# Routing rounds by six digit steps in place of nine, with equal keys settled by running counts

## The chip, the cores and the metric

The kernel runs on one core of a Trainium2 chip, in one launch, in fp32 at its inputs and its output. The time is the device time in microseconds of that core; the number given for a kernel is the median over its runs. A core has five engines that work side by side: TensorE (PE in the profile) for matrix products, VectorE (DVE) and ScalarE (ACT) for elementwise work, GpSimd (POOL), and SyncE (SP), which starts transfers.

## The reference

Three stages follow one another on 2304 tokens of 512 values: attention, a routed layer with eight experts, and a rational function between two matrix products. The routing is the part of interest:

```python
def _moe_ref(x, w_gate, w1, w2):
    ...
    cap = N // E                      # 288
    logits = x @ w_gate               # 2304 x 8
    order = np.argsort(-logits.flatten())
    ...
    for idx in order:
        tok, e = (int(idx) // E, int(idx) % E)
        if assigned[tok] >= 0 or counts[e] >= cap:
            continue
        assigned[tok] = e
        counts[e] += 1
    ...
        h = np.maximum(x[mask] @ w1[e], 0.0)
        out[mask] = h @ w2[e]
```

Pairs of a token and an expert are taken in falling order of their logit, each token once, until an expert has 288 tokens. Each expert's network then runs on its own 288 tokens.

## The kernel before

The tokens lie as 128 partitions by NT = 17 columns, so that `logit` is 128 x 17 x 8. Attention fills `logit` in its last part. The routing (`routing_dve`, `routing_pe`) is a loop of seven rounds, written with `Fori(0, E - 1)`, and a pass behind it for the tokens that are left. In each round every free token has a best open expert (`choice`, one-hot) and a `key`, its logit there. At least one expert is closed in each round: the round looks for the largest key at which some open expert has as many tokens at or above it as it still has places (`need8`), and gives these tokens away.

The key is searched by digits, from the highest. A float key is turned into an integer in the same order (`flip`, L777 to L781), cut into seven digits (L772), and the token's number, in three more digits of which one is shared with the key's last bits, makes all keys different; these are nine digits `digit[:, 0:9, :]`, with 32 values each and 16 in the last. A digit step is:

- VectorE compares `y`, the scaled remainder of the key, with the values 1 to k of `kval`: `ge`, 128 x k x 18 in bf16, in two halves of 10 and 8 columns (L805).
- TensorE counts: for each of the 17 columns, a product of `choice` (128 x 8, the weights) with `ge[:, 0:k, t]` (128 x k, read with a stride of 18 elements), added up in `pO` (L862). The first half of `ge` releases ten of the products, the second seven.
- Beside it VectorE makes `w` and `z`, the next remainder (L808, L811).
- VectorE compares the counts with `need8`: `sat`, 8 x k (L815). TensorE adds up `sat` over the experts: `pX` (L865). VectorE counts the values with a sum above 0.5: `found`, the digit (L818), and makes the next `y` from `z` and `found` (L821).

Behind the last step VectorE marks the tokens at or above the key (`took`, L822; `new`, L823), sums them by expert (`newsum`, L827), updates `free` and `owner`, TensorE adds the sums over the partitions in two products (L867, L868), and VectorE updates `room`, `closed` and `need8` (L832 to L838). The next round begins with `opened` (L736), `keys` (L733), `is_best` (L740), then `ranked`, `first_rank`, `is_first` (L744 to L751), which leave the first of several equal experts, and `chosen` (L755).

The order on an engine is the order of the program. `do` counts an instruction on the semaphore `s_rt`, `after(k)` makes VectorE wait for the k-th, and `link` does both at once: a linked instruction ends before the next starts.

```python
                def link(ins):
                    after(do(ins))
```

GpSimd works beside the routing: it subtracts the high parts of `w_in` and `w_out` from their originals (L919, four instructions of 2048 elements each, as soon as transfers have landed) and does the same with the first expert's weights (L1028). Then it waits for `slot`, the place of each token, and scatters the tokens' rows to memory, sorted by expert (L885, 17 indirect transfers). SyncE loads the first expert's rows behind that, and the experts' part begins. Ahead of everything, `routing_setup_pool` and `routing_setup_dve` make the constants; VectorE's attention work stands behind the latter.

## Time and profile before

| | us |
|---|---|
| time, median of 3 runs | 1251.15 (1249.8 to 1251.74) |
| the profiled execution | 1253.45 |
| its span, first to last instruction | 1251.6 |
| attention, to the last logit | 0 to 279 |
| routing, to the last `slot` | 279 to 523 |
| scatter, loads and first products | 523 to 560 |
| experts and rational function | 560 to 1252 |
| PE / DVE / ACT / POOL busy in the span | 965.1 / 792.7 / 506.8 / 244.9 |

The profile is of one execution, and its own time is 1.85 us above its span. The granted TensorE clock is 0.9 of full speed in the attention and the experts' part and 0.5 in the routing. In the timelines a row gives the start and the length in us, the engine, the line, the operation with output and inputs, and in brackets the idle time ahead of it and what ended it. An instruction's length includes the time that it stands still for a resource. Successive instructions of an engine overlap a little, by some 0.08 us on VectorE.

### The profile page before, as it was taken

How to read it: one execution, taken by the hardware profiler on the slowest of the kernel's cores; microseconds unless marked ns; L12 is line 12 of the kernel's file. 1: busy time of each engine (PE TensorE's matmuls, PEld its weight loads, DVE VectorE, ACT ScalarE, POOL GpSimd, SP SyncE). 2: the span in 40 equal slices, each digit the busy share in tenths (PEclk: the TensorE clock that was granted, in tenths of full speed). 3: DMA queues.
4: the chain of work that ended last, by engine and by line, in shares of the span. 5: the costliest groups of instructions: out<-in, count | busy, mean ns of one | idle time of the engine just before them, and what ended most of it. 6: DMA issues, size and time to landing. Idle time of an engine off the chain costs nothing.

```text
span 1251.6 us, 22365 instructions
## 1 busy us (share of the span) xinstructions
PE 965.1 (77%) x7769; PEld 895.3 (72%) x7769; DVE 792.7 (63%) x1757; ACT 506.8 (40%) x1108; POOL 244.9 (20%) x199
## 2 busy tenths in 40 slices
PE   5999999972133444219899898998998988989994
PEld 4888888851123333219899898998998988988994
DVE  4555554438876666403975966939849759488484
ACT  3555555520010000003744735627547457266362
POOL 2000000005530000230421412313215114132101
PEclk9999999975555555559999999999999999999998
DMA  7622222204320000135015024051060240420200
GB/s 224 191 64 64 64 64 64 46 11 134 135 67 0 0 0 0 52 130 154 1 39 132 0 75 96 0 135 36 17 154 0 67 103 0 110 61 0 69 1 18
DMA packets 106280, 80.62 MB, mean 64 GB/s; under 512 B 72016, under 2 KB 88400, under 8 KB 105232
## 3 DMA queue, kind: packets, MB, share of 16 engines
q1 hardware_dynamic: 97184, 62.83, 19.1%
q0 software_dynamic: 9072, 17.47, 4.5%
q8 instruction: 15, 0.25, 0.1%
q14 instruction: 9, 0.07, 0.0%
HBM read 70.94 MB, written 9.31 MB: 64 GB/s over the span
## 4 chain that ended last, share of the span: by engine, by line
PE 51%; DVE 35%; issue 7%; ACT 3%; POOL 2%; DMA 1%; DVEq 0%; ACTq 0%; SPq 0%; POOLq 0%
PE pS L1095 6%; PE pS L1097 6%; PE pS L1096 6%; DVE num L1351 6%; DVE num L1353 6%; PE pO L862 5%; PE pS L339 4%; DVE den L1340 3%; DVE num L1344 3%; PE pO L362 3%; DVE ge L805 2%; PE pO L363 2%; DVE num L1342 2%; DVE den L1349 2%; DVE z L811 2%
## 5 line engine op out<-in xcount | busy, mean ns | idle before, releaser
L1028 POOL TENSOR_TENSOR w_lo<-w_raw,w_hi 128x512 fp32r<-128x512 f32 x80 | 129.8, 1643 | 290.8 <-ACT w_hi L1023 290.8
L1023 ACT ACTIVATE w_hi<-w_raw 128x512 fp32r<-128x512 f32 x80 | 45.5, 616 | 275.9 <-DMA w_raw<-in_moe_w 275.9
L1095 PE MATMUL pS<-x_hi,win_hi 128*128 128x272 f32 x512 | 149.2, 292 | 4.5 <-DVE num L1344 4.5
L862 PE MATMUL pO<-ge,choice 128*8 128x32 bf16 (+1 forms) x1071 | 71.1, 233 | 101.6 <-DVE ge L805 101.6
L1097 PE MATMUL pS<-x_hi,win_lo 128*128 128x272 f32 x512 | 148.0, 289 | 0.0
L1096 PE MATMUL pS<-x_lo,win_hi 128*128 128x272 f32 x512 | 147.9, 289 | 0.0
L862 PEld LDWEIGHTS pO<-ge,choice 128*8 128x8 bf16 x1071 | 59.2, 102 | 108.5 <-DVE ge L805 108.5
L1095 PE MATMUL pT<-g_hi,wout_hi 128*128 128x272 f32 x256 | 79.5, 310 | 47.0 <-DVE g_lo L1331 47.0
L1095 PEld LDWEIGHTS pS<-x_hi,win_hi 128*128 128x128 f32 x512 | 96.4, 188 | 6.6 <-DVE num L1344 6.3
L1096 PEld LDWEIGHTS pS<-x_lo,win_hi 128*128 128x128 f32 x512 | 96.4, 188 | 0.0
L1097 PEld LDWEIGHTS pS<-x_hi,win_lo 128*128 128x128 f32 x512 | 96.3, 188 | 0.0
L1095 PEld LDWEIGHTS pT<-g_hi,wout_hi 128*128 128x128 f32 x256 | 49.8, 195 | 55.0 <-issue 54.6
L1351 DVE SCALAR_TENSOR_TENSOR num<-num,coef,habs 128x544 f32<-128x544 f32 x64 | 86.1, 1345 | 0.0
L1353 DVE SCALAR_TENSOR_TENSOR num<-den,num 128x544 f32<-128x544 f32 x64 | 80.4, 1256 | 2.2
L1395 POOL DMA_INDIRECT out<-orow,number x32 | 37.6, 1175 | 214.2 <-DVE orow L1375 206.8
L485 ACT ACTIVATE prob<-pS,negmax 128x224 f32<-128x224 f32 x128 | 55.8, 444 | 55.9 <-DVE negmax L521 55.4
L1095 PE MATMUL pS<-x_hi,w_hi 128*128 128x272 f32 x256 | 76.1, 297 | 1.2 <-POOL w_lo L1028 1.2
L1096 PE MATMUL pT<-g_lo,wout_hi 128*128 128x272 f32 x256 | 75.6, 295 | 0.0
L1097 PE MATMUL pT<-g_hi,wout_lo 128*128 128x272 f32 x256 | 75.5, 295 | 0.0
L1097 PE MATMUL pS<-x_hi,w_lo 128*128 128x272 f32 x256 | 75.1, 293 | 0.0
L1258 ACT ACTIVATE g_hi<-num 128x544 fp32r<-128x544 f32 x64 | 42.3, 660 | 80.9 <-DVE num L1353 76.3
L1096 PE MATMUL pS<-x_lo,w_hi 128*128 128x272 f32 x256 | 74.9, 292 | 0.0
(222 smaller groups left out, 2851.8 us busy)
## 6 DMA issues: line engine op xcount, KB each, us to landing
...
```

The costliest lines, as they stand in the source:

```text
L339: last = nc.tensor.matmul(bank[:, h * KW:(h + 1) * KW], qT[par][:, h, i * P:(i + 1) * P], kT[par][:, i, :], start=False, stop=True, skip_g ...
L485: e = nc.scalar.activation(prob[:, i, h, :], pS[:, i * 512 + h * KW:i * 512 + (h + 1) * KW], ACT.Exp, bias=negmax[par][:, c:c + 1], accum_ ...
L862: last = nc.tensor.matmul(pO[0:E, 0:k], choice[:, t, :], ge[:, 0:k, t], start=t == 0, stop=t == NT - 1)
L1023: nc.scalar.activation(piece(w_hi, slot, k % 2), piece(w_raw, slot, k % 2), ACT.Copy).then_inc(s_whi, 1)
L1028: nc.gpsimd.tensor_tensor(piece(w_lo, slot, k % 2), piece(w_raw, slot, k % 2), piece(w_hi, slot, k % 2).bitcast(F32), ALU.subtract).then_i ...
L1095: nc.tensor.matmul(dst, hi, x_hi, start=start, stop=False)
L1096: nc.tensor.matmul(dst, hi, x_lo, start=False, stop=False)
L1097: return nc.tensor.matmul(dst, lo, x_hi, start=False, stop=stop)
L1258: nc.scalar.activation(g_hi[k % 2][:, :, :], num[k % 2][:, :, :], ACT.Copy).then_inc(s_gh, 1)
L1351: nc.vector.scalar_tensor_tensor(n, n, coef[:, 0:1], r, ALU.add, ALU.mult).then_inc(s_ratio, 1)
L1353: nc.vector.scalar_tensor_tensor(n, d, 2.0, n, ALU.subtract, ALU.mult).then_inc(s_g, 1)
L1395: nc.gpsimd.indirect_dma_start(out, bass.IndirectOffsetOnAxis(number[:, s:s + 1].bitcast(U32), 0), orow[s][:, :], None).then_inc(s_send, 16)
```

## The change

The key is cut into six digits, of 64, 64, 32, 32, 32 and 32 values, and the token's number is no longer part of it. `y` is fp32 in place of bf16 and always scaled by 64; with it `z` needs one addition (the passes `w` are gone). Keys can now be equal at the end. So each round marks the tokens above the key (`above`) and those equal to it (`tied`), both in `won`, laid out by expert; TensorE makes the sum of those above, the sum of all, and, with the triangular matrix `before`, how many equal ones lie in lower partitions, in five products; a running count over each expert's columns (`tensor_tensor_scan` into `spot`) then says which of the equal ones still find a place. Another running count (`count`) finds the first of several equal experts of a token, in place of `ranked`, `first_rank` and `is_first`. The token's being free comes from `owner` (`holding`, `lifted`) in place of `free`. `kval` has 64 values in place of 32. The experts' and the attention's parts are untouched.

```diff
-        KG = 32
-        DIGITS = [(27, 31), (22, 31), (17, 31), (12, 31), (7, 31), (2, 31), (0, 3)]
-        LD = len(DIGITS)
-        KS = [KG] * 8 + [16]
-        ND = len(KS)
-        IDMAX = 4095
+        DIGITS = [(26, 63), (20, 63), (15, 31), (10, 31), (5, 31), (0, 31)]
+        KS = [m + 1 for _, m in DIGITS]
+        ND = len(DIGITS)
+        KG = max(KS)
+        RADIX = float(KG)
         ABOVE = 1e6
...
-        took = sb("took", [P, NT], BF16)
-        new = sb("new", [P, NT, E], BF16)
-        newsum = sb("newsum", [P, E], BF16)
+        y = sb("y", [P, NT + 1])
+        won = sb("won", [P, 2, E, NT + 1])
+        wonsum = sb("wonsum", [P, 2, E], BF16)
...
-            nc.gpsimd.iota(erank[:, :], pattern=[[-1, E]], base=E, channel_multiplier=0,
-                           allow_small_or_imprecise_dtypes=True).then_inc(s_const, 1)
+            nc.gpsimd.memset(fresh_e[:, :, :], 1.0).then_inc(s_const, 1)
...
-        TSETUP = 13
+        TSETUP = 9
...
-            link(nc.vector.tensor_scalar(flip[:, :], token[:, :], -1.0, float(IDMAX), ALU.mult, ALU.add))
-            link(nc.vector.tensor_scalar(tokbits[:, 0, :], flip[:, :], 9, None, ALU.logical_shift_right))
-            link(nc.vector.tensor_scalar(tokbits[:, 1, :], flip[:, :], 4, 31, ALU.logical_shift_right, ALU.bitwise_and))
-            link(nc.vector.tensor_scalar(tokbits[:, 2, :], flip[:, :], 15, None, ALU.bitwise_and))
-            link(nc.vector.memset(dconst[:, :, :], 1 / KG))
-            link(nc.vector.tensor_scalar(dconst[:, LD - 1:ND, :], tokbits[:, :, :], 1.0, 1 / KG, ALU.add, ALU.mult))
+            link(nc.vector.memset(fresh_e[:, :, 0:1], 0.0))
+            link(nc.vector.memset(fresh_t[:, :, :], 1.0))
+            link(nc.vector.memset(fresh_t[:, :, 0:1], 0.0))
             link(nc.vector.memset(y[:, :], 0.0))
-            link(nc.vector.tensor_copy(digit[:, LD:ND, :], dconst[:, LD:ND, :]))
-            link(nc.vector.memset(free[:, :], 1.0))
+            link(nc.vector.memset(won[:, :, :, :], 0.0))
             link(nc.vector.memset(room[:, :], float(CAP)))
             link(nc.vector.memset(closed[:, :], 0.0))
             link(nc.vector.memset(room8[:, :], float(CAP)))
             link(nc.vector.memset(need8[:, :], float(CAP)))
...
+            def holding():
+                return nc.vector.tensor_reduce(out=held[:, :], in_=owner[:, :, :], axis=AX, op=ALU.add)
+
+
+            def lifted():
+                return nc.vector.scalar_tensor_tensor(lift[:, :], held[:, :], -FULL, key[:, :], ALU.mult, ALU.add)
+
...
-                                               key[:, :].unsqueeze(2).to_broadcast([P, NT, E]), ALU.is_equal)
...
+                                               lift[:, :].unsqueeze(2).to_broadcast([P, NT, E]), ALU.is_equal)
+
+
+            def counted():
+                return nc.vector.tensor_tensor_scan(count[:, :, :].rearrange("p t e -> p (t e)"),
+                                                    fresh_e[:, :, :].rearrange("p t e -> p (t e)"),
+                                                    best[:, :, :].rearrange("p t e -> p (t e)"), 0.0, ALU.mult, ALU.add)
 
             def chosen():
-                return nc.vector.tensor_tensor(choice[:, :, :], best[:, :, :],
-                                               free[:, :].unsqueeze(2).to_broadcast([P, NT, E]), ALU.mult)
+                return nc.vector.scalar_tensor_tensor(choice[:, :, :], count[:, :, :], 1.0, best[:, :, :], ALU.is_equal,
+                                                      ALU.mult)
...
-                link(opened())
...
+                    shift, m = DIGITS[j]
+                    return nc.vector.tensor_scalar(digit[:, j, :].bitcast(I32), flip[:, :], shift, m, ALU.logical_shift_right,
+                                                   ALU.bitwise_and)
+
+                k_open = do(opened())
+                k_held = do(holding())
+                after(k_open)
+                k_key = do(keys())
+                after(k_key)
                 k_sign = do(nc.vector.tensor_scalar(flip[:, :], bits, 31, -2 ** 31, ALU.arith_shift_right, ALU.bitwise_or))
-                after(k_best)
-                k_ranked = do(ranked())
+                k_lift = do(lifted())
                 after(k_sign)
                 k_flip = do(nc.vector.tensor_tensor(flip[:, :], bits, flip[:, :], ALU.bitwise_xor))
-                after(k_ranked)
-                k_rank = do(first_rank())
+                after(k_lift)
+                k_best = do(is_best())
                 after(k_flip)
-                do(cut(0))
-                do(cut(1))
-                after(k_rank)
-                k_first = do(is_first())
-                do(cut(2))
-                do(cut(3))
-                after(k_first)
+                for j in range(3):
+                    do(cut(j))
+                after(k_best)
+                k_count = do(counted())
+                for j in range(3, ND):
+                    k_cut = do(cut(j))
+                after(k_count)
                 do(chosen())
-                do(cut(4))
-                do(cut(5))
-                link(cut(6))
-                link(nc.vector.scalar_tensor_tensor(digit[:, 0:LD, :], dbits[:, :, :], 1 / KG, dconst[:, 0:LD, :], ALU.mult,
-                                                    ALU.add))
-
-
-
-                link(nc.vector.tensor_scalar(y[:, 0:NT], digit[:, 0, :], float(KG), None, ALU.mult))
+                after(k_cut)
+                link(nc.vector.tensor_scalar(digit[:, :, :], digit[:, :, :].bitcast(I32), 1 / RADIX, 1 / RADIX, ALU.mult, ALU.add))
+
+
+
+                link(nc.vector.tensor_scalar(y[:, 0:NT], digit[:, 0, :], RADIX, None, ALU.mult))
                 for j in range(ND):
                     k = KS[j]
                     for t0, t1 in ((0, HALF), (HALF, NT + 1)):
                         nc.vector.tensor_tensor(ge[:, 0:k, t0:t1], y[:, t0:t1].unsqueeze(1).to_broadcast([P, k, t1 - t0]),
                                                 kval[:, 0:k, t0:t1], ALU.is_ge).then_inc(s_ge, 1)
-                    if j > 0:
-                        link(nc.vector.tensor_scalar(w[:, :], z[:, :], found[:, :], None, ALU.subtract))
-                    y_now = w[:, :] if j > 0 else digit[:, 0, :]
                     if j < ND - 1:
-                        link(nc.vector.scalar_tensor_tensor(z[:, :], y_now, float(KG), digit[:, j + 1, :], ALU.mult, ALU.add))
-                    else:
-                        link(nc.vector.tensor_scalar(z[:, :], y_now, float(KG), None, ALU.mult))
+                        link(nc.vector.tensor_tensor(z[:, :], y[:, 0:NT], digit[:, j + 1, :], ALU.add))
                     dve.wait_ge(s_cnt, ph * ND + (j + 1))
...
                     link(nc.vector.tensor_scalar(anyk[:, 0:k], pX[:, 0:k], 0.5, None, ALU.is_gt, ALU.add,
                                                  accum_out=found[:, :]))
                     if j < ND - 1:
-                        link(nc.vector.tensor_scalar(y[:, 0:NT], z[:, :], found[:, :], float(KG), ALU.subtract, ALU.mult))
-                link(nc.vector.scalar_tensor_tensor(took[:, :], z[:, :], found[:, :], free[:, :], ALU.is_ge, ALU.mult))
-                link(nc.vector.tensor_tensor(new[:, :, :], choice[:, :, :], took[:, :].unsqueeze(2).to_broadcast([P, NT, E]),
-                                             ALU.mult))
-
+                        link(nc.vector.tensor_scalar(y[:, 0:NT], z[:, :], found[:, :], RADIX, ALU.subtract, ALU.mult))
+                    else:
+                        link(nc.vector.tensor_scalar(z[:, :], y[:, 0:NT], found[:, :], None, ALU.subtract))
+
+
+                past = z[:, :].unsqueeze(2).to_broadcast([P, NT, E])
+                above = won[:, 0, :, 1:NT + 1].rearrange("p e t -> p t e")
+                tied = won[:, 1, :, 1:NT + 1].rearrange("p e t -> p t e")
+                k_above = do(nc.vector.scalar_tensor_tensor(above, past, 0.5, choice[:, :, :], ALU.is_gt, ALU.mult))
+                k_tied = do(nc.vector.scalar_tensor_tensor(tied, past, 0.0, choice[:, :, :], ALU.is_equal, ALU.mult))
+                after(k_tied)
                 with nc.allow_low_precision("counts up to NT"):
-                    nc.vector.tensor_reduce(out=newsum[:, :], in_=new[:, :, :].rearrange("p t e -> p e t"), axis=AX,
-                                            op=ALU.add).then_inc(s_took, 1)
-                do(nc.vector.tensor_tensor(free[:, :], free[:, :], took[:, :], ALU.subtract))
-                do(nc.vector.tensor_tensor(owner[:, :, :], owner[:, :, :], new[:, :, :], ALU.add))
+                    nc.vector.tensor_reduce(out=wonsum[:, :, :], in_=won[:, :, :, 1:NT + 1], axis=AX, op=ALU.add)\
+                        .then_inc(s_took, 1)
+                k_owner = do(nc.vector.tensor_tensor(owner[:, :, :], owner[:, :, :], above, ALU.add))
                 dve.wait_ge(s_count, ph + 1)
-                k_room = do(nc.vector.tensor_tensor(room[:, :], room[:, :], pT[0][:, 0:E], ALU.subtract))
+                k_lim = do(nc.vector.tensor_tensor(won[:, 1, :, 0], pT[0][:, 0:E], room[:, :], ALU.subtract))
+                after(k_lim)
+                k_scan = do(nc.vector.tensor_tensor_scan(spot[:, :, :].rearrange("p e t -> p (e t)"),
+                                                         fresh_t[:, :, :].rearrange("p e t -> p (e t)"),
+                                                         won[:, 1, :, :].rearrange("p e t -> p (e t)"), 0.0, ALU.mult, ALU.add))
+                k_room = do(nc.vector.tensor_tensor(room[:, :], room[:, :], pT[0][:, E:2 * E], ALU.subtract))
                 k_room8 = do(nc.vector.tensor_tensor(room8[:, :], room8[:, :], pT[1][0:E, 0:1], ALU.subtract))
+                after(k_scan)
+                k_new = do(nc.vector.scalar_tensor_tensor(tied, spot[:, :, 1:NT + 1].rearrange("p e t -> p t e"), 0.5, tied,
+                                                          ALU.is_lt, ALU.mult))
                 after(k_room)
                 do(nc.vector.tensor_scalar(closed[:, :], room[:, :], 0.5, FULL, ALU.is_lt, ALU.mult))
                 after(k_room8)
-                link(nc.vector.tensor_scalar(need8[:, :], room8[:, :], 0.5, ABOVE, ALU.is_lt, ALU.mult))
+                k_need = do(nc.vector.tensor_scalar(need8[:, :], room8[:, :], 0.5, ABOVE, ALU.is_lt, ALU.mult))
+                after(k_new)
+                do(nc.vector.tensor_tensor(owner[:, :, :], owner[:, :, :], tied, ALU.add))
+                after(k_need)
                 link(nc.vector.tensor_tensor(need8[:, :], need8[:, :], room8[:, :], ALU.add))
                 assert step[0] == STEPS, step[0]
...
-            for stage_of in (opened, keys, is_best, ranked, first_rank, is_first, chosen):
+            link(opened())
+            link(holding())
+            for stage_of in (keys, lifted, is_best, counted, chosen):
                 link(stage_of())
...
-                nc.tensor.matmul(pT[0][:, 0:E], ones[:, :], newsum[:, :], start=True, stop=True)
-                nc.tensor.matmul(pT[1][0:E, 0:1], newsum[:, :], ones[:, 0:1], start=True, stop=True).then_inc(s_count, 1)
+                above, tied = wonsum[:, 0, :], wonsum[:, 1, :]
+                nc.tensor.matmul(pT[0][:, 0:2 * E].rearrange("p (a e) -> p a e", a=2), ones[:, :],
+                                 above.unsqueeze(1).to_broadcast([P, 2, E]), start=True, stop=False)
+                nc.tensor.matmul(pT[0][:, 0:E], before[:, :], tied, start=False, stop=False)
+                nc.tensor.matmul(pT[0][:, E:2 * E], ones[:, :], tied, start=False, stop=True)
+                nc.tensor.matmul(pT[1][0:E, 0:1], above, ones[:, 0:1], start=True, stop=False)
+                nc.tensor.matmul(pT[1][0:E, 0:1], tied, ones[:, 0:1], start=False, stop=True).then_inc(s_count, 1)
```

## Rows read from the trace of the kernel before

**Rows 1.** Windows, one routing round each: busy time and count of each engine, clock, DMA.
```profile
279.44:324.58 45.14, 12.37 (x164) 9.51 (x164) 34.45 (x98) 0.00 (x0) 19.27 (x5) 0.50 0.54 176
324.58:375.28 50.70, 12.37 (x164) 9.51 (x164) 42.02 (x99) 4.60 (x8) 28.09 (x12) 0.50 0.15 51
375.28:403.85 28.57, 12.21 (x164) 9.54 (x164) 17.88 (x98) 0.00 (x0) 0.00 (x0) 0.50 0.00 0
```

**Rows 2.** Timeline, GpSimd, 350 to 525 us: start, length, engine, line, operation; then idle.
```profile
523.20 1.07 POOL L885 DMA_INDIRECT x_by_expert<-x_sb,slot  x1 [162.82 <-DVE slot L852]
```

**Rows 3.** Timeline, one digit step with 32 values, 409 to 413 us.
```profile
409.68 0.53 DVE L805 TENSOR_TENSOR ge<-y,kval 128x320 bf16<-128x320 bf16 x2
...
410.06 1.18 PE L862 MATMUL pO<-ge,choice 128*8 128x32 bf16 x17 [0.93 <-DVE ge L805]
...
411.27 0.24 DVE L815 TENSOR_SCALAR sat<-pO,need 8x32 bf16<-8x32 f32 x1 [0.70 <-PE pO L862]
...
412.04 0.24 DVE L821 TENSOR_SCALAR y<-z,found 128x17 bf16<-128x17 f32 x1
412.31 0.53 DVE L805 TENSOR_TENSOR ge<-y,kval 128x320 bf16<-128x320 bf16 x2
```

**Rows 4.** Timeline, last step, tail and next head, 428 to 436 us.
```profile
428.18 0.38 DVE L805 TENSOR_TENSOR ge<-y,kval 128x160 bf16<-128x160 bf16 x2
...
428.48 0.69 PE L862 MATMUL pO<-ge,choice 128*8 128x16 bf16 x17 [0.85 <-DVE ge L805]
...
429.21 0.22 DVE L815 TENSOR_SCALAR sat<-pO,need 8x16 bf16<-8x16 f32 x1 [0.29 <-PE pO L862]
...
429.94 0.24 DVE L822 SCALAR_TENSOR_TENSOR took<-z,found,free 128x17 bf16<-128x17 f32 x1
...
430.55 0.39 DVE L827 TENSOR_REDUCE newsum<-new 128x8 bf16<-128x136 bf16 x1
...
430.99 0.19 PE L867 MATMUL pT<-newsum,ones 128*128 128x8 bf16 x1 [1.31 <-DVE newsum L827]
...
431.11 0.17 PE L868 MATMUL pT<-ones,newsum 128*8 128x1 bf16 x1
431.32 0.16 DVE L832 TENSOR_TENSOR room<-room,pT 128x8 f32<-128x8 f32 x1 [0.16 <-PE pT L868]
...
432.42 0.30 DVE L736 TENSOR_TENSOR open_logit<-logit,closed 128x136 f32<-128x136 f32 x1 [0.48 <-DVE need L838]
...
435.60 0.53 DVE L805 TENSOR_TENSOR ge<-y,kval 128x320 bf16<-128x320 bf16 x2
```

**Rows 5.** Instructions by shape, 403.8 to 432.42 us: count, busy us, mean ns.
```profile
L805 DVE TENSOR_TENSOR ge<-y,kval 128x320 bf16<-128x320 bf16 x8 | 2.6, 325 | 0.3
...
L736 DVE TENSOR_TENSOR open_logit<-logit,closed 128x136 f32<-128x136 f32 x2 | 0.6, 301 | 1.0 <-DVE need L838 1.0
...
L805 DVE TENSOR_TENSOR ge<-y,kval 128x160 bf16<-128x160 bf16 x1 | 0.2, 243 | 0.0
```

**Rows 6.** Line 1353 over the whole span: duration ns shortest, median, longest.
```profile
L1353 DVE SCALAR_TENSOR_TENSOR num<-den,num x64: 724/1685/1709, 595.0 to 1229.7; 128x544 f32<-128x544 f32 x64
```

**Rows 7.** Timeline of the start, 0 to 11 us.
```profile
5.07 1.18 POOL L660 IOTA kval<- 128x576 bf16 x1
...
7.35 0.40 DVE L695 TENSOR_SCALAR flip<-token 128x17 int32<-128x17 int32 x1 [1.19 <-POOL token L671]
...
10.04 0.69 DVE L509 COPY kT<-pX 128x512 f32<-128x512 f32 x1
```

**Rows 8.** Timeline, GpSimd's three bursts, and a VectorE instruction against the second.
```profile
294.91 18.07 POOL L919 TENSOR_TENSOR win_lo<-stage,win_hi 128x2048 fp32r<-128x2048 f32 x4 [14.22 <-DMA wout_hi<-in_moe_w_out]
328.08 18.07 POOL L919 TENSOR_TENSOR wout_lo<-stage,wout_hi 128x2048 fp32r<-128x2048 f32 x4 [15.10 <-DMA stage<-in_moe_w_out]
350.36 10.02 POOL L1028 TENSOR_TENSOR w_lo<-w_raw,w_hi 128x512 fp32r<-128x512 f32 x8 [4.21 <-ACT w_hi L1023]
...
328.21 17.98 DVE L811 SCALAR_TENSOR_TENSOR z<-digit 128x17 f32<-128x17 f32 x1
```

49 lines of the change are left out of this document (18 added, 31 removed).

## The prediction

> **What bounds the kernel now.** I read the windows by routing round first, then one round in order of time, then the same instructions grouped by shape, and last GpSimd's queue. The windows show seven rounds. From the third on they are alike, 28.57 us each at a granted clock of 0.50, which is the 1.2 GHz level; the first takes 45.14 and the second 50.70 [rows 1]. Nothing else of weight runs in the quiet ones: the loop is one chain that goes back and forth between VectorE and TensorE, so what is saved in it comes off the span. That the chain leads to the end is seen on GpSimd: its first scatter starts after 162.82 us idle, released by `slot`, the routing's result [rows 2]. The scatter, the load of the sorted rows and the experts stand behind it and would move with it as a block.
>
> A step with 32 values reads as follows [rows 3]: `ge` starts at 409.68, TensorE at 410.06, `sat` at 411.27, `y` at 412.04, the next `ge` at 412.31. A round's eight such steps take 21.15 us, from the first `ge` (a round ahead of the one at 435.60, so at 407.03) to the last step's at 428.18 [rows 4], hence 2.64 each. The last step, with 16 values, takes 1.76 (428.18 to 429.94), the tail behind it 2.48 (to 432.42), the head before the next `ge` 3.18 (to 435.60). Together 28.57.
>
> **Prices.** `ge` of 320 and 160 bf16 elements takes 325 and 243 ns, 0.51 ns per element and 161 fixed; an fp32 operation on 136 takes 301, so 1.03 per element with the same fixed part [rows 5]. From TensorE's start to `sat` it is 1.21 us with 32 columns [rows 3] and 0.73 with 16 [rows 4]: 0.48 for each 16 columns of the 17 products. From `sat` to `y` [rows 3], or to `took` [rows 4], it is 0.77 and 0.73, so 0.04 per 16. Reading with a stride of eight elements, `newsum` takes 0.39 us for 136 [rows 4] against 0.30 in order: 0.66 ns more for each element out of order.
>
> **The digit steps.** `y` becomes fp32, and with one fp32 operand I expect `ge` at the fp32 rate: 491 ns for 320 elements, +0.17; 820 for 640, +0.50. The second half of `ge` stays beside TensorE's first ten products and costs nothing; its cover is about 0.6 us, and the half ends some 0.3 (32 values) or 0.55 (64) behind TensorE's start, ahead of the eleventh product. Both ends of the fp32 price: none of it (+0 and +0.17), or as taken. `w` goes, but it lay beside the products: nothing. A step with 32 values comes to 2.81. One with 64 adds 0.50, 0.96 (32 more columns) and 0.08 to 2.64: 4.18. Six steps are 2 x 4.18 + 4 x 2.81 = 19.60, where nine were 21.15 + 1.76 = 22.91: -3.31 a round. The 0.96 is a line through two sizes. Its low end is one column per cycle of 1.2 GHz, 32 x 17 x 0.83 = 0.45; its high end is that all of the 1.21 doubles. I take the line, since 16 and 32 both lie on it and the stride in `ge` stays the same.
>
> **The head.** Out go `ranked`, `first_rank`, `is_first` and the joining pass; in come `holding` (0.30, under `opened` for a third), `lifted` (a small one, 0.18) and a scan over 136 elements; the cuts fill gaps as before. No scan stands in the trace. It does two dependent operations for each element, so its ends are one such operation (0.30) and two in a row (0.60); I take 0.44, the fixed part and twice the stream. Placed one behind the other with the distances of [rows 4] (a waited 0.30 operation costs 0.33, an unwaited one 0.22, a small one 0.11 to 0.20), the chain `opened`, `holding`, `key`, `lifted`, `best`, three cuts, scan, three cuts, `choice`, `digit`, `y` is 2.86 instead of 3.18: -0.32.
>
> **The tail.** `above` and `tied` write with a stride of 18 words: 0.45 each with `newsum`'s surcharge, the second 0.37 behind the first. With `tied` waited for, the sum over 272 elements (0.44) starts at 0.84, and TensorE at 1.33. There were two products 0.12 apart and 0.33 from the first to `room` [rows 4]; there are five, so +0.28: 0.61, and the small difference starts at 1.94. The scan over 144 waits for that one (0.20) and takes 0.46. Then `tied` is cut back (0.45 with a strided read and write, at 2.73), `closed` and `need` lie beside it, `owner` takes the ties in (start at 3.30, 0.39), the last `need` starts at 3.61, and the next round 0.63 behind it: 4.21 in place of 2.48, **+1.73**. The new wait for five products holds nothing back but this chain; `owner` += `above` lies under it.
>
> Ends of the unknown prices: three strided passes between 0.30 and 0.55 each, two scans between 0.30 and 0.60: -0.7 to +0.6 a round.
>
> Two pages speak against me here. L1353, a scalar_tensor_tensor with two fp32 inputs in SBUF, takes 724 ns for 544 elements at its shortest [rows 6], which is 1.03 each, full rate. The Trainium skill (Vector Engine (DVE) Microarchitecture Reference, section 7) says that this shape halves the throughput. The trace disagrees with it; by that rule `choice` and the cut-back `tied` would cost 0.28 a round more, 2 us in all. For a write stepping 24 words at each element the same page (section 5.2) gives 2.5 ns per element; no row of the trace has such a write, and by that figure the three strided passes would cost some 0.3 a round more, again 2 us. By the Trainium skill (DVE: opcode table, instruction layouts, handler registers and perf-mode slots, section 6) the scan runs at half throughput, which would be 0.44 and 0.46.
>
> **Sum.** -3.31 - 0.32 + 1.73 = -1.90 a round, 26.67 in place of 28.57; seven rounds -13.3. The pass behind the loop trades four waited operations for four of the same size: 0. At the start, GpSimd's `kval` list doubles (1.18 us for 576 elements, so +1.2) and VectorE's setup waits for that queue; but the setup chain from 7.35 to 10.04 [rows 7] shrinks from thirteen links to nine short ones, by about as much: 0, within 0.5.
>
> **GpSimd's bursts.** The first two rounds cost 16.57 and 22.13 us more than a quiet one: 38.7. GpSimd subtracts for 18.07 us from 294.91, for 18.07 from 328.08 and for 10.02 from 350.36, and VectorE's `z`, 17 elements, stands 17.98 us against the second [rows 8]. The bursts hang on transfers and on one another, not on the rounds, so they stay where they are. The new rounds meet them at 4.2- or 2.8-us steps that hold `ge`, `ge`, `z` and `y` of the same kinds, so something is caught within a step. The first burst would meet the new fourth step, 1.1 us ahead of its `y`; the second the first step of the second round. I take 38.7 again. All three bursts last 46.2, so it can rise by 7.5 at most; slipping between more of GpSimd's instructions could save some 5.
>
> The profiled execution has 1253.45 with a span of 1251.6; it becomes 1240.2. The median of the runs shown, 1251.15, lies 2.3 below it: **1238**.
>
> **The rivals.**
> *Cheap columns.* The two sizes don't make a line; more columns cost a cycle each, and the strided passes cost less. 0.51 less on each wide step is 1.02 a round, 7 us: 1230. For it speaks the stretch from `sat` to `y`: three operations whose columns lie in order, and 0.04 us more for all of them with 16 more. Against it: `ge` is read with a stride, and there 16 more columns cost 0.48 over 17 products, 1.8 for each.
> *Gains given back in the bursts.* All of the 7.5 is lost again: 1245. Against it: `z` already stands the whole of the second burst.
> *The tail eats it (slower).* The settlement of equal keys is serial and runs in every round, ties or not. About 960 elements pass on its path. At 2.0 ns more for each, three times what I took for a stream in order, 1.90 a round is gone; at 2.5 more it is 1255. For it: five of the passes are of kinds or strides that no row shows. Against it: the strided row pays 0.66.
> *Nothing moves.* The rounds lie behind something else: no row does that, since GpSimd idles for `slot`.
>
> **How the numbers follow.** As forecast 0.60 (1233 to 1243), cheap columns 0.17, given back in the bursts 0.15, tail slower 0.04, no change 0.04. The range 1229 to 1247 leaves out the last two and the corners. A measurement here tells 0.2% (2.5 us) from no change: faster 0.92, same 0.04, slower 0.04.
>
> **What would show it.** A quiet round of 26.7; wide steps of 4.2 and narrow ones of 2.8; `ge` at 491 and 820 ns; scans near 0.45; 4.2 from the last `z` to `opened`; the first two rounds together 38 to 40 above two quiet ones; the span from `slot` to the end unchanged. The forecast is wrong if wide steps exceed 5.0, if the tail passes 5.5, or if the experts' part changes.

## The result

The changed kernel takes 1229.3 us (median; 1228.68 to 1232.94), the kernel before beside it 1250.47 (1248.28 to 1251.74): a ratio of 0.984, with an interval of 0.981 to 0.986. The forecast was 1238 in a range of 1229 to 1247, faster with a chance of 0.92. So the direction was right, and the gain was 21 us, 1.6%, where 13 were forecast. 1229.3 lies 0.3 us inside the low end of the range. In its profiled execution the changed kernel takes 1232.94 with a span of 1231.2, where before it was 1253.45 and 1251.6, so 20.4 less.

### Where the time went

The windows by routing round of the changed kernel, then the same view for the whole span cut at the first `open_logit` and at the first scatter (columns: stretch and its length, busy us and count of PE, PEld, DVE, ACT and POOL, then the granted clock, the DMA share and GB/s):

```profile
279.42:321.12 41.70, 10.78 (x113) 8.12 (x113) 32.73 (x71) 0.00 (x0) 19.49 (x5) 0.50 0.50 153
321.12:367.25 46.13, 11.10 (x113) 7.97 (x113) 39.61 (x71) 4.59 (x8) 29.65 (x12) 0.50 0.25 90
367.25:393.19 25.94, 10.63 (x113) 8.16 (x113) 16.30 (x71) 0.00 (x0) 0.00 (x0) 0.50 0.00 0
```

```profile
279.42:502.01 222.59, 76.23 (x808) 58.01 (x808) 157.25 (x509) 4.59 (x8) 49.14 (x18) 0.50 0.15 47
502.01:1231.20 729.19, 630.51 (x4864) 619.66 (x4864) 491.36 (x672) 372.71 (x648) 179.92 (x136) 0.95 0.23 62
```

A quiet round takes 25.94 where it took 28.57 [rows 1]: 2.63 less, and there are 113 products in it for 164. The clock is 0.50 as before. The first round falls from 45.14 to 41.70, the second from 50.70 to 46.13. From the first `open_logit` to the first scatter it was 523.20 - 279.44 = 243.76 [rows 1, 2]; it is 222.59 now, 21.17 less. In front of it nothing moved (279.44 to 279.42), behind it 1251.6 - 523.20 = 728.4 became 729.19. So the routing carries all of the difference: seven rounds' worth of 2.63 is 18.4, and the other 2.7 lie in the two rounds under GpSimd's bursts.

GpSimd still idles for `slot`, now 140.36 us instead of 162.82 [rows 2]. The timeline of GpSimd in the changed kernel (start, length, engine, line, operation, idle before):

```profile
502.01 1.07 POOL L893 DMA_INDIRECT x_by_expert<-x_sb,slot  x1 [140.36 <-DVE slot L855]
```

One step with 64 values, from the timeline of the changed kernel at 374 us, to be laid beside [rows 3]:

```profile
374.18 1.43 DVE L795 TENSOR_TENSOR ge<-y,kval 128x640 bf16<-128x640 f32 x2
...
375.06 2.14 PE L865 MATMUL pO<-ge,choice 128*8 128x64 bf16 x17 [1.46 <-DVE ge L795]
...
377.24 0.27 DVE L800 TENSOR_SCALAR sat<-pO,need 8x64 bf16<-8x64 f32 x1 [1.54 <-PE pO L865]
...
378.37 0.83 DVE L795 TENSOR_TENSOR ge<-y,kval 128x320 bf16<-128x320 f32 x2
```

From `ge` to the next `ge` it is 4.19; from TensorE's start to `sat` 2.18. The four narrow steps take 2.80 or 2.81. The settlement behind the last step, from the same view:

```profile
389.59 0.39 DVE L814 SCALAR_TENSOR_TENSOR won<-z,choice 128x136 f32<-128x136 f32 x1
389.83 0.38 DVE L815 SCALAR_TENSOR_TENSOR won<-z,choice 128x136 f32<-128x136 f32 x1
390.24 0.44 DVE L818 TENSOR_REDUCE wonsum<-won 128x16 bf16<-128x272 f32 x1
...
390.73 0.19 PE L871 MATMUL pT<-wonsum,ones 128*128 128x16 bf16 x1 [1.68 <-DVE wonsum L818]
...
390.93 0.16 PE L876 MATMUL pT<-ones,wonsum 128*8 128x1 bf16 x1
391.13 0.17 DVE L822 TENSOR_TENSOR won<-pT,room 128x8 f32<-128x8 f32 x1 [0.16 <-PE pT L876]
391.34 0.46 DVE L824 TENSOR_TENSOR_SCAN spot<-fresh_t,won 128x144 f32<-128x144 bf16 x1
...
391.84 0.38 DVE L830 SCALAR_TENSOR_TENSOR won<-spot,won 128x136 f32<-128x136 f32 x1
...
392.27 0.37 DVE L837 TENSOR_TENSOR owner<-owner,won 128x136 bf16<-128x136 bf16 x1
...
393.19 0.30 DVE L727 TENSOR_TENSOR open_logit<-logit,closed 128x136 f32<-128x136 f32 x1 [0.49 <-DVE need L839]
```

From the first masking pass (389.59) to the next round's `open_logit` (393.19) it is 3.60. The same instructions by shape in one quiet round (count, busy us, mean ns), which answer to [rows 5]:

```profile
L795 DVE TENSOR_TENSOR ge<-y,kval 128x320 bf16<-128x320 f32 x4 | 2.0, 492 | 0.1
...
L795 DVE TENSOR_TENSOR ge<-y,kval 128x640 bf16<-128x640 f32 x2 | 1.7, 826 | 0.1
...
L746 DVE TENSOR_TENSOR_SCAN count<-fresh_e,best 128x136 f32<-128x136 bf16 x1 | 0.4, 432 | 0.0
...
L751 DVE SCALAR_TENSOR_TENSOR choice<-count,best 128x136 bf16<-128x136 f32 x1 | 0.3, 292 | 0.0
```

And GpSimd's bursts, with what VectorE does under the second one, which answer to [rows 8]:

```profile
295.21 18.28 POOL L927 TENSOR_TENSOR win_lo<-stage,win_hi 128x2048 fp32r<-128x2048 f32 x4 [14.52 <-DMA wout_hi<-in_moe_w_out]
327.43 18.93 POOL L927 TENSOR_TENSOR wout_lo<-stage,wout_hi 128x2048 fp32r<-128x2048 f32 x4 [13.94 <-DMA stage<-in_moe_w_out]
```

```profile
327.78 4.18 DVE L806 TENSOR_SCALAR y<-z,found 128x17 f32<-128x17 f32 x1
331.99 10.00 DVE L795 TENSOR_TENSOR ge<-y,kval 128x640 bf16<-128x640 f32 x2
341.91 4.49 DVE L798 TENSOR_TENSOR z<-y,digit 128x17 f32<-128x17 f32 x1
```

The bursts have kept their place and length (18.28 from 295.21, 18.93 from 327.43). What stands in them has changed: before, one `z` of 17 elements stood 17.98 us against all four instructions of the second burst [rows 8]; now `y` takes 4.18, the two halves of `ge` 10.00 together and `z` 4.49. That is about one GpSimd instruction (18.93 / 4 = 4.7 us) for each of the four.

### The profile page after: what moved, and what is told of

Read it like the earlier page. It is cut to its first block, busy times and chain, and to the rows that moved or that the text cites. A ratio compares the mean times of both kernels' runs of the same rounds, so it can differ in the third digit from the quotient of the medians.

```text
span 1231.2 us, 21262 instructions
## 1 busy us (share of the span) xinstructions
PE 956.8 (78%) x7412; PEld 888.5 (72%) x7412; DVE 779.6 (63%) x1564; ACT 507.5 (41%) x1108; POOL 248.0 (20%) x199
## 4 chain that ended last, share of the span: by engine, by line
PE 45%; DVE 25%; issue 19%; DMA 4%; POOL 4%; ACT 3%; DVEq 0%; SPq 0%; ACTq 0%; POOLq 0%
PE pS L1103 6%; PE pS L1105 6%; PE pS L1104 6%; DVE num L1359 6%; DVE num L1361 6%; PE pS L339 4%; DVE den L1348 4%; DVE num L1352 3%; PE pO L362 3%; PE pO L363 2%; DVE num L1350 2%; DVE den L1357 2%; POOL wout_lo L927 2%; PE pX L329 1%; PE pT L422 1%
## 5 line engine op out<-in xcount | busy, mean ns | idle before, releaser
L865 PE MATMUL pO<-ge,choice 128*8 128x32 bf16 (+1 forms) x714 | 63.6, 256 | 106.3 <-DVE ge L795 106.3
L865 PEld LDWEIGHTS pO<-ge,choice 128*8 128x8 bf16 x714 | 51.0, 103 | 114.1 <-DVE ge L795 112.0
L1103 PE MATMUL pT<-g_hi,wout_hi 128*128 128x272 f32 x256 | 80.1, 313 | 44.6 <-DVE g_lo L1339 44.6
## 6 DMA issues: line engine op xcount, KB each, us to landing
wout_hi<-in_moe_w_out POOLq DMA_DIRECT2D x1, 4096.0 KB, 15.6
```

The source lines that it names most:

```text
L865: last = nc.tensor.matmul(pO[0:E, 0:k], choice[:, t, :], ge[:, 0:k, t], start=t == 0, stop=t == NT - 1)
L1103: nc.tensor.matmul(dst, hi, x_hi, start=start, stop=False)
```

## Experiments

All of them change the changed kernel, at one or two places, and are timed beside the kernel before. They were timed in several groups, in which the kernel before had medians from 1250.4 to 1253.6, so times of different groups are compared by their ratios; the changed kernel's own is 0.984 [0.981, 0.986].

### The changed kernel once more

> The changed kernel once more, unedited, as a second sample of how its first two rounds meet GpSimd's bursts. Theory (how many VectorE instructions slip between GpSimd's is a matter of chance from execution to execution): quiet rounds of 25.94 again, the first two rounds together within 86 to 91, the time 1228 to 1233. Rival (the first rounds are fixed): 87.8 to 0.2.

1234.0 us, ratio 0.985 [0.983, 0.987]. The quiet rounds are 25.93 again, the first two 42.84 and 46.15. So the extra time under the bursts was 37.1 here, 36.0 in the first profile. This is the scatter against which small differences in that term are to be read. The median is 4.7 us above the first one, 2.6 of which the kernel before shows as well (1253.04 for 1250.47).

### `y` in bf16 again

```diff
-        y = sb("y", [P, NT + 1])
+        y = sb("y", [P, NT + 1], BF16)
```

> The changed kernel with y in bf16 in place of fp32; nothing else. Theory (the comparison ge is paid at the fp32 rate): ge of 640 and 320 elements falls from 0.82 and 0.49 us to 0.49 and 0.33, wide steps from 4.19 to 3.69, narrow ones from 2.80 to 2.64, a quiet round from 25.94 to 24.3, the time from 1229 to about 1217.5. Rival (the extra length of ge lies beside TensorE's products): the round stays at 25.9 and the time at 1229.

1226.5 us, ratio 0.979 [0.978, 0.981]. By shape, one round of this kernel:

```profile
L795 DVE TENSOR_TENSOR ge<-y,kval 128x320 bf16<-128x320 bf16 x4 | 1.3, 325 | 0.1
...
L795 DVE TENSOR_TENSOR ge<-y,kval 128x640 bf16<-128x640 bf16 x2 | 1.0, 491 | 0.1
```

`ge` falls from 826 to 491 ns and from 492 to 325. So the price of the fp32 remainder was as forecast: 0.33 for each wide half on the path and 0.17 for each narrow one, 1.34 a round by the rows and 1.30 by the rounds (25.93 to 24.63). The expectation's 3.69 for a wide step was a slip of mine, since 0.33 was to be taken off and not 0.50; it measures 3.86. Seven rounds give 9.1 us, and the bursts took back 2.9 (38.9 extra against 36.0), so that the routing of the profiled execution is 6.2 shorter (222.59 to 216.42); the ratios say 0.5%, or 5.9 us. Nothing is lost in bf16: where the higher digits match, `y` is a whole number from 1 to 64. The fp32 remainder costs 1.3 us a round and buys nothing here.

### Seven narrower digits instead of six

```diff
-        DIGITS = [(26, 63), (20, 63), (15, 31), (10, 31), (5, 31), (0, 31)]
+        DIGITS = [(27, 31), (22, 31), (17, 31), (12, 31), (7, 31), (2, 31), (0, 3)]
```

> The changed kernel with seven digits, six of 32 values and one of 4, in place of six with two of 64; y stays fp32. Theory (a wide step costs 1.39 us more than a narrow one and the seventh, of 4 values, some 1.7): the steps take 6 x 2.80 + 1.7 = 18.5 in place of 19.6, a round 24.9, the time about 1222. Rival (what counts is the number of steps, as the change supposes): a seventh step adds 1.7 and the wide ones gave nothing away, a round of 27 and a time of 1238 or more.

1226.9 us, ratio 0.979 [0.977, 0.981]. Little of that is the routing's: of the 5.4 us by which the profiled execution is shorter (1231.2 to 1225.8), 3.5 lie ahead of the first `open_logit`, where nothing was changed, and 1.9 in the routing, since the bursts cost 40.2 here and took back 4.2. The rows tell more. A quiet round takes 25.06, so 0.88 less: six steps of 2.80 and a last one of 1.84 make 18.64, where the six steps of the change make 19.61. The timeline of its last step, which has four values:

```profile
436.30 0.59 PE L865 MATMUL pO<-ge,choice 128*8 128x4 bf16 x17 [0.80 <-DVE ge L795]
436.93 0.21 DVE L800 TENSOR_SCALAR sat<-pO,need 8x4 bf16<-8x4 f32 x1 [0.58 <-PE pO L865]
```

With 4 columns it is still 0.63 from TensorE's start to `sat`. In the trace's single records these 17 products start 26.6 ns apart, and each is recorded with 168 ns, so that 16 distances and the last product make the 0.59: here fewer columns no longer bring the products closer together. A step costs by its fixed part and by its columns, and with columns at their price in this layout a 64-value step is no good trade: 4.19 for six bits is 0.70 a bit, 2.80 for five bits 0.56.

### The layout of `ge`

```diff
-        ge = sb("ge", [P, KG, NT + 1], BF16)
+        ge = sb("ge", [P, NT + 1, KG], BF16)
...
-                        nc.vector.tensor_tensor(ge[:, 0:k, t0:t1], y[:, t0:t1].unsqueeze(1).to_broadcast([P, k, t1 - t0]),
-                                                kval[:, 0:k, t0:t1], ALU.is_ge).then_inc(s_ge, 1)
+                        nc.vector.tensor_tensor(ge[:, t0:t1, 0:k], y[:, t0:t1].unsqueeze(2).to_broadcast([P, t1 - t0, k]),
+                                                kval[:, t0:t1, 0:k], ALU.is_ge).then_inc(s_ge, 1)
...
-                        last = nc.tensor.matmul(pO[0:E, 0:k], choice[:, t, :], ge[:, 0:k, t], start=t == 0, stop=t == NT - 1)
+                        last = nc.tensor.matmul(pO[0:E, 0:k], choice[:, t, :], ge[:, t, 0:k], start=t == 0, stop=t == NT - 1)
```

`kval` and its iota turn in the same way.

> The changed kernel with ge and kval laid out column by column of tokens, so that TensorE reads the 32 or 64 values in order in place of with a stride of 18. Theory (the stride makes a column cost 1.77 ns in place of 0.83): from TensorE's start to sat 2.18 falls to about 1.2 with 64 values and 1.21 to 0.7 with 32, a round loses about 4 us, the time falls to about 1200. Rival (the products are paced by their weight loads, one for each product): no change in the round, 1229.

1204.2 us, ratio 0.961 [0.959, 0.963]: the largest single step on the routing that keeps all of its work (222.59 to 197.80 us in the profiles). A wide and a narrow step of this kernel, from its timeline:

```profile
430.97 1.13 PE L865 MATMUL pO<-ge,choice 128*8 128x64 bf16 x17 [5.70 <-DVE ge L795]
...
432.14 0.27 DVE L800 TENSOR_SCALAR sat<-pO,need 8x64 bf16<-8x64 f32 x1 [0.54 <-PE pO L865]
```

```profile
419.69 0.69 PE L865 MATMUL pO<-ge,choice 128*8 128x32 bf16 x17 [1.08 <-DVE ge L795]
...
420.41 0.24 DVE L800 TENSOR_SCALAR sat<-pO,need 8x32 bf16<-8x32 f32 x1 [0.35 <-PE pO L865]
```

From TensorE's start to `sat` it is 1.17 with 64 columns, where it was 2.18, and 0.72 with 32, where it was 1.22. Between the two sizes lie 32 columns of 17 products, 544 in all. In the change they cost 0.96, so 1.77 ns a column; in order they cost 0.45, so 0.83 ns, one column per cycle of 1.2 GHz. The single records say the same without the ends of the row: the products start 117 and 60 ns apart in the change (64 and 32 columns), 53 and 26.6 in order. The last of these is also the distance of the products with 4 columns above. The clock is 0.50 in both, and `ge`'s own write is as fast (826 and 492 ns in both layouts). So it was the read of `ge` with a step of 36 bytes that doubled the price of a column. The faster products have brought out a wait that the forecast had rightly put at nothing for the old layout: the eleventh product now stands for the second half of `ge`, 0.15 us behind the tenth with 64 columns and 0.10 with 32. The wide steps lose 1.0 each, the narrow ones 0.49, together 3.96, and the quiet round falls by 3.99, to 21.95. The Trainium skill (SBUF — State Buffer, section "Door 1: The DMA port swizzle") says that reads which leave a 16-byte line at every element pay a penalty, so that bf16 can step only within 8 elements for free; the two layouts agree with it, and give its size here, 0.94 ns a column at the 1.2 GHz level.

### Both together

> The changed kernel with both y in bf16 and the order of ge by token columns. y is then read with a step of 0 along the innermost axis. Theory (the bf16 rate holds for it too): ge of 640 and 320 falls from 0.82 and 0.49 us to 0.49 and 0.33, a quiet round from order's 21.94 to 20.6. Rival (the double rate needs both inputs to advance, as choice<-best,free and new<-choice,took, both with a repeated input, suggest at 0.30 us for 136): 21.9, as order.

The two edits above in one kernel: 1205.9 us, ratio 0.965 [0.963, 0.966], and a quiet round of 22.00, so no gain over the layout alone. By shape:

```profile
L795 DVE TENSOR_TENSOR ge<-y,kval 128x320 bf16<-128x320 bf16 x14 | 6.9, 492 | 0.5
...
L795 DVE TENSOR_TENSOR ge<-y,kval 128x640 bf16<-128x640 bf16 x6 | 5.0, 826 | 0.2
```

All operands are bf16, and `ge` still takes 826 and 492 ns. In this layout one element of `y` is repeated along the innermost direction; in the other one the innermost direction walks over `y`. The double rate of [rows 5] goes with the walk as well as with the type. The two savings exclude one another, and 0.5 us per step from the columns is worth more than 0.17 or 0.33 from `ge`.

### Without the settlement of equal keys

```diff
-                k_above = do(nc.vector.scalar_tensor_tensor(above, past, 0.5, choice[:, :, :], ALU.is_gt, ALU.mult))
-                k_tied = do(nc.vector.scalar_tensor_tensor(tied, past, 0.0, choice[:, :, :], ALU.is_equal, ALU.mult))
-                after(k_tied)
+                k_above = do(nc.vector.scalar_tensor_tensor(above, past, -0.5, choice[:, :, :], ALU.is_gt, ALU.mult))
+                after(k_above)
...
-                nc.tensor.matmul(pT[0][:, 0:E], before[:, :], tied, start=False, stop=False)
-                nc.tensor.matmul(pT[0][:, E:2 * E], ones[:, :], tied, start=False, stop=True)
```

The small difference, the scan, the cut-back and the second pass on `owner` go as well.

> The changed kernel without the settlement of equal keys: all tokens at or above the key are taken, with one sum over 136 elements, two products and no scan over tied, no cut-back and one update of owner. Left out: that an expert stops at its last place among equal keys. Theory (the settlement is what the tail grew by): from the last z to the next round's start 3.60 falls to about 2.2, a round to 24.5, the time to about 1219.5. Rival (the tail is mostly fixed hand-offs): 0.4 a round at most, 1226.

1223.8 us, ratio 0.977 [0.975, 0.979]. From the masking pass to `open_logit`, on the timeline:

```profile
438.25 0.39 DVE L813 SCALAR_TENSOR_TENSOR won<-z,choice 128x136 f32<-128x136 f32 x1
...
440.45 0.30 DVE L727 TENSOR_TENSOR open_logit<-logit,closed 128x136 f32<-128x136 f32 x1 [0.49 <-DVE need L827]
```

From the first masking pass (438.25) to `open_logit` it is 2.20 instead of 3.60, and the quiet round falls by 1.41 to 24.53. The settlement is thus 1.4 a round, 9.9 us of the whole. The shorter row of steps saved 3.30 a round, so the trade is a good one, but two fifths of what it brought go to the settlement, and in every round.

### GpSimd's subtractions in smaller pieces

```diff
-        PART = 2048
+        PART = 512
```

and the same with 256. The first two bursts then are 16 or 32 instructions each, over the same data.

> The changed kernel with GpSimd's subtractions of the two weight matrices cut into pieces of 512 elements in place of 2048, thus 32 instructions of about 1.15 us in place of 8 of 4.5. Theory (a VectorE instruction that meets GpSimd's waits for the end of one instruction, not of the burst; in the third burst, of 512-element pieces, a step takes 5.3 us in place of 2.8): the two bursts of 18 us lose about 9 each in place of 16, the first two rounds together fall from 87.8 to about 74, the time to about 1217. Rival (VectorE stands still for as long as GpSimd has work queued): the first two rounds stay at 88, the time at 1231.

> As part512, with pieces of 256 elements. Theory (the wait is one GpSimd instruction, here about 0.6 us, but GpSimd's fixed time grows and it must win the port 64 times): the first two rounds fall a little further, to about 70, the time to about 1213. Rival of part512: 88 and 1231. A third case: GpSimd's bursts stretch by what VectorE takes, so that this equals part512.

1221.0 us, ratio 0.977 [0.976, 0.979], and 1216.7, ratio 0.973 [0.971, 0.975]. With 512, GpSimd's burst and what VectorE does under it:

```profile
293.95 1.15 DVE L806 TENSOR_SCALAR y<-z,found 128x17 f32<-128x17 f32 x1
295.13 2.90 DVE L795 TENSOR_TENSOR ge<-y,kval 128x320 bf16<-128x320 f32 x2
297.95 1.24 DVE L798 TENSOR_TENSOR z<-y,digit 128x17 f32<-128x17 f32 x1
```

The bursts themselves grow longer, from 18.3 us to 21.0 and 25.3. VectorE's instructions wait less all the same: `y` stands 1.15 us, the two `ge` 2.90, `z` 1.24, a GpSimd instruction of 1.3 us for each of the four, and between GpSimd's instructions VectorE gets its turn. The first two rounds together take 73.5 and 64.0 us, where 74 and 70 were expected, against 87.8. But the third burst, of 512 elements in all kernels so far, slips from the second round to the third, with 256 the end of the second burst too, and this costs there (30.5 and 36.2 us for 25.9). The time lost in the rounds under the bursts is 36.0 us at 2048, 26.2 at 512 and 22.4 at 256. So in these kernels it isn't the length of the burst that VectorE pays but that of the instruction that holds it, once for each instruction of VectorE that meets one. It is no upper bound: in the kernel before, `z` stood against four GpSimd instructions of 4.5 us in a row [rows 8]. Why it got no turn between them is open.

### A GpSimd that only writes

```diff
-                    nc.gpsimd.tensor_tensor(l[:, part], stage[:, part], h[:, part].bitcast(F32), ALU.subtract)\
-                        .then_inc(s_lo, 1)
+                    nc.gpsimd.memset(l[:, part].bitcast(F32), 0.0).then_inc(s_lo, 1)
```

The low parts of the first two weights are left out in this kernel (they are zero).

> The changed kernel with GpSimd writing zeros to win_lo and wout_lo in place of subtracting; left out are the low parts of the two matrices, so the last two products lose their correction terms. Theory (VectorE's stalls in the first two bursts come from sharing GpSimd's way to SBUF for reading): with writes alone ge and z pass; what remains is y, a one-input instruction that wrote 3.55 us late in the first burst, and the third burst, which is untouched. The first two rounds together take 52 to 62 in place of 87.8, the time is 1195 to 1205. Rival (the transfers or the writes slow VectorE, reads or not): at least 75.

1205.6 us, ratio 0.962 [0.960, 0.964]. GpSimd's first burst and VectorE under it:

```profile
295.00 7.10 POOL L927 MEMSET win_lo<- 128x2048 f32 x4 [14.19 <-DMA wout_hi<-in_moe_w_out]
```

```profile
296.87 0.83 DVE L795 TENSOR_TENSOR ge<-y,kval 128x320 bf16<-128x320 f32 x2
297.61 0.17 DVE L798 TENSOR_TENSOR z<-y,digit 128x17 f32<-128x17 f32 x1
...
299.40 0.95 DVE L806 TENSOR_SCALAR y<-z,found 128x17 f32<-128x17 f32 x1
```

While GpSimd writes (295.00 to 302.10), `ge` takes 0.83 for both halves and `z` 0.17, as in a quiet round; `y` alone is late, 0.95 for 0.24, and under the second burst once 1.87. The first round costs 27.28, 1.34 more than a quiet one; the second, in which the third burst still subtracts, 33.68. So two causes are apart here: the length of the burst, and the reads. With 7.1 us the writing burst is shorter than the 18.3 of the reading one, but a `ge` that passes unhindered under it shows that reads are what stands against instructions with two inputs in SBUF. The Trainium skill (SBUF — State Buffer, section "Who interferes with whom") says that such an instruction contends with a GpSimd instruction that reads SBUF, not with one that only writes it; `ge` and `z` agree, in both kernels. That `y` is held up by a GpSimd that only writes is another matter: the same section of the page says that a tensor_scalar within SBUF, which `y` is, can run in a mode that takes both of VectorE's port pairs and then contends with GpSimd in any case. That would fit. It also fits that the sum `wonsum`, which has one input as well but is no tensor_scalar, takes 0.44 us in the midst of a subtracting burst (at 308.47 in the kernel with pieces of 512), as in a quiet round. But no run here tells it from another cause. The first two rounds come to 60.96 against 87.83 in the change.

### Layout and pieces together

> The changed kernel with order's layout and part256's pieces. Theory (the two savings lie in different places, TensorE's products and VectorE's stalls): quiet rounds of 21.95, the first three rounds 13 us shorter than order's 105, the time about 1191. Rival (part of the bursts' cost was hidden behind the longer products): half of it, 1198.

> As order_part256 with pieces of 128 elements. Theory (GpSimd's fixed time grows faster than VectorE's waits shrink: 128 instructions, bursts of some 32 us each): within 3 us of order_part256, either way. Rival (the wait for one GpSimd instruction is all that counts): 6 us less than order_part256.

1194.6 us, ratio 0.953 [0.951, 0.955], and 1188.4, ratio 0.949 [0.947, 0.950]. The first kernel falls between its two expectations, 1191 and 1198: its first three rounds are 15.7 us shorter than those of the layout alone, where 13 were expected, but the third burst now reaches into the fourth, which takes 27.2 for 21.9. The rounds of the second are 24.10, 27.59, 24.92, 32.99 and then 21.94: the bursts now last 32 us each, reach into the fourth round, and cost 21.8 in all, where they cost 39.1 with this layout and pieces of 2048. Down to 128 elements the shorter instruction wins over the longer burst. That speaks for the rival in the expectation, by which only the wait for a single GpSimd instruction counts: 6 us less than 1194.6 was its forecast.

### The third kind of piece

In round four stand, behind the end of the second burst, 10.7 us of subtractions of 512 elements each. They are made by the routine that also works all through the experts' part. The last kernel cuts it as well, on top of the one before:

```diff
-            nc.gpsimd.tensor_tensor(piece(w_lo, slot, k % 2), piece(w_raw, slot, k % 2),
-                                    piece(w_hi, slot, k % 2).bitcast(F32), ALU.subtract).then_inc(s_wlo, 1)
+            for i in range(4):
+                part = slice(i * 128, (i + 1) * 128)
+                low = nc.gpsimd.tensor_tensor(piece(w_lo, slot, k % 2)[:, part], piece(w_raw, slot, k % 2)[:, part],
+                                              piece(w_hi, slot, k % 2)[:, part].bitcast(F32), ALU.subtract)
+            low.then_inc(s_wlo, 1)
```

> order_part128 with the subtraction of the experts' weights cut as well, four instructions of 128 elements for each of 512, in the routing's third burst and in all of the experts' part. Theory (a stall costs only where the chain passes: in the routing the third burst's cost of about 5 us halves; in the experts' part TensorE is busy 630 of 719 us and VectorE's stalled num has some slack): 1188 becomes 1182 to 1186. Rival (the two num instructions, 1.0 us longer than they need be in 54 of 64 turns, hold TensorE up each time): 1140 to 1150. Third case (GpSimd, made slower by the fixed cost of each piece, delays the weights): slower than 1188.

1148.7 us, ratio 0.917 [0.915, 0.918]: 8.3% below the kernel before, and 6.6% below the change. The rival's time came true: the routing gave about 2 us of what was left in the bursts, and the experts' part gave the rest. The windows from the first scatter to the end, without and with the cut:

```profile
457.00:1185.50 728.50, 630.10 (x4864) 619.16 (x4864) 491.29 (x672) 372.73 (x648) 179.75 (x136) 0.95 0.23 62
```

```profile
456.90:1150.70 693.80, 615.85 (x4864) 608.22 (x4864) 453.43 (x672) 371.24 (x648) 262.44 (x352) 0.96 0.24 65
```

The experts' part falls from 728.50 to 693.80. In it VectorE's busy time falls by 38 us, though not an instruction of it has changed (672 in both), and GpSimd's rises by 83. One line of VectorE in both (shortest, median and longest ns), and the products that wait for VectorE:

```profile
L1361 DVE SCALAR_TENSOR_TENSOR num<-den,num x64: 724/1679/1709, 528.6 to 1163.4; 128x544 f32<-128x544 f32 x64
```

```profile
L1364 DVE SCALAR_TENSOR_TENSOR num<-den,num x64: 724/866/876, 528.9 to 1128.6; 128x544 f32<-128x544 f32 x64
```

```profile
L1103 PE MATMUL pT<-g_hi,wout_hi 128*128 128x272 f32 x256 | 80.2, 313 | 44.7 <-DVE g_lo L1339 44.6
```

```profile
L1106 PE MATMUL pT<-g_hi,wout_hi 128*128 128x272 f32 x256 | 75.9, 297 | 24.3 <-DVE g_lo L1342 24.3
```

The median of this instruction falls from 1679 to 866 ns; unhindered it is 724 in both. It was held in 35 of its 64 runs (not in 54, as the expectation has it), and so was the other long `num` in the same 35 turns; the GpSimd instructions of the experts' part have a mean of 1.68 us, and of 0.74 with the cut. TensorE's idle time for `g_lo` falls from 44.6 to 24.3.

That is 20.4 of the 34.7 us by which the experts' part is shorter, since TensorE's whole idle time falls by as much (98.4 to 78.0). The other 14.2 are TensorE's busy time, for the same 4864 products, and here the granted clock comes in. Two stretches without the cut, and nearly all of the part with it:

```profile
705.00:710.30 5.30, 2.33 (x19) 2.13 (x18) 5.23 (x7) 3.82 (x7) 1.86 (x3) 1.00 0.00 0
710.50:713.70 3.20, 3.20 (x15) 3.20 (x15) 3.17 (x3) 1.99 (x4) 3.16 (x2) 0.50 0.00 0
```

```profile
499.80:1141.30 641.50, 607.56 (x4822) 600.07 (x4821) 451.50 (x667) 368.15 (x640) 241.16 (x325) 1.00 0.24 61
```

Without the cut the granted clock fell to 0.50, the 1.2 GHz level, for seven short stretches between 539 and 1056 us, 24 us together. Ahead of each TensorE had stood still for a good part of the time, as in the first of these rows, where it was busy for 2.33 of 5.30 us. With the cut it did not fall once between 500 and 1141. That the shorter waits kept the clock up is argued from this, not tested by a run of its own. The 103 products in the seven stretches take 0.23 us each, where those at the full clock take 0.13, so some 10 of the 14.2 us are theirs, an estimate from these rows. So the rival's reason, that VectorE's stalls hold TensorE up, gives 20 us directly, and its time was met because TensorE's busy time fell as well, of which it says nothing.

The chain of work that ended last says what bounds the kernel; first without, then with the cut:

```profile
PE 46%; DVE 26%; issue 13%; POOL 6%; ACT 4%; DMA 4%; DVEq 0%; SPq 0%; ACTq 0%; POOLq 0%
```

```profile
PE 63%; issue 12%; DVE 9%; POOL 6%; ACT 4%; DMA 4%; SPq 0%; DVEq 0%; ACTq 0%; POOLq 0%
```

## Why the prediction was right, and by how much it was off

*What bounds the kernel.* Held. The routing is one chain, what was saved in it came off the span, and `slot` to the end moved by 0.8 us.

*The digit steps.* Held to a hundredth in sum: 19.61 (369.98 to 389.59) against 19.60. Wide 4.19 and narrow 2.80 against 4.18 and 2.81; `ge` 826 and 492 ns against 820 and 491; TensorE's part of a wide step 2.18, which is 1.21 and the 0.96 of the line through two sizes. The rival *cheap columns* (0.45) fell, as its counter-argument said: `ge` is read with a stride. Its time of 1230 is nearer to the measured 1229.3 than the forecast of 1238 is, but by luck: the wide steps took 4.19, not the 3.67 that it needs, and the difference came from other terms. `order` shows that the counter-argument was the right one, since without the stride the rival's 0.45 is what is measured. What I didn't draw from it is that the dearer column is no price of the step but of the layout.

*The head.* 2.73 (367.25 to 369.98) against 2.86. The scan over 136 elements takes 432 ns (forecast 0.44), the one over 144 takes 457 (0.46), which is twice the stream of an ordinary pass; the Trainium skill (DVE: opcode table, instruction layouts, handler registers and perf-mode slots, section 6) gives half throughput, and the rows agree. `choice` takes 292 ns with two fp32 inputs, so the rule on that shape (Vector Engine (DVE) Microarchitecture Reference of the Trainium skill, section 7), which would have made it 0.44, is not borne out here either.

*The tail.* This is the term that was mis-sized: 3.60 against 4.21. Counted from the first masking pass, the second starts 0.24 behind it and not 0.37, the sum at 0.65 and not 0.84, TensorE at 1.14 and not 1.33: 0.19. The small difference starts 0.40 behind TensorE and not 0.61, another 0.21: the four further products of 1 to 8 columns start 0.20 in all behind the first (390.73 to 390.93), 0.05 each, and the reader starts 0.40 behind the first, where two products had taken 0.33. Three more products thus cost 0.07, and I had added 0.28 for them. The scan and the distance to the cut-back give 0.08, the cut-back 0.14. The strided passes take 386, 380 and 383 ns, not 450. Part of that was no matter of the chip: `newsum`'s surcharge, 90 ns on 136 elements [rows 4], added to 301 ns makes 0.39, and I wrote 0.45. Against 301 in order it is 0.62 ns more for each element that steps 18 words. The Trainium skill (Vector Engine (DVE) Microarchitecture Reference, section 5.2) has 2.50 ns at a step of 24 words against 1.05 in order, which would be 1.5 more; no run here has that step. The estimate that I hung on this figure, 0.3 a round above the sum, was wrong too: 136 times the page's 2.5 and the fixed 161 ns [rows 5] make an estimate of 0.50 a pass, 0.05 above the 0.45 in the sum, so 0.15 a round. The item "4.2 from the last `z` to `open_logit`" was moreover put loosely: the sum counts from the masking pass; from `z` (389.32) it is 3.87.

*The bursts.* 36.0 against 38.7. The mechanism of the forecast (something is always caught) held, and the size is a matter of what is caught. Over seven profiles with pieces of 2048 it came out at 36.0 and 37.1 (the change), 37.5 (both edits together), 38.7 (no settlement), 38.9 (`y` in bf16), 39.1 (layout) and 40.2 (seven digits), so 38.7 was a fair middle, and plus or minus 3 would have been its honest bound. That the first profile fell at the low end of these, 2.7 under the forecast, is chance as far as these runs tell; the median of the kernel timed once more, 1234.0, lies nearer to 1238. The rival *given back in the bursts* didn't come about.

*The sum.* The quiet round came out at 25.94 and not 26.67, 0.73 less: 0.13 of it in the head, 0.61 in the tail. Seven times that is 5.1; the bursts give 2.7; together 7.8 of the 8.7 between 1238 and 1229.3. The rest is within what two medians differ by. Both errors pointed the same way, and together they used up nearly the whole lower side of the range. The tail's alone is within the -0.7 to +0.6 a round given for its unknown prices, though a third of it (0.21) came from the products, which were not among these. The start was forecast at 0 and moved by 0.02. The rival *the tail eats it* would have needed 2.0 ns more for each of some 960 elements; it was 0.62 on the strided ones.

What stays open: why `y` waits for a writing GpSimd, and why `z` got no turn between four GpSimd instructions in the kernel before. That pieces of 128 in the experts' part brought 34.7 us there in the profiles and 39.7 between the medians (1188.4 to 1148.7) needs no cause: the profiled execution without the cut was the fastest of its four (1187.26), the one with it the slowest (1152.48). The stretch ahead of the first `open_logit` took between 276.0 and 279.6 us over the kernels, though nothing in it was changed; that is why the rounds and not the ends are compared above, and its cause is open. Whether seven digits in the in-order layout would do as well as six wasn't tried; by its rows six times 2.31 and one of 1.84 make 15.7, as against 2 x 3.19 + 4 x 2.31 = 15.6, so it would be level.
